# Attention, gated MLP and routed experts on one core: where the softmax is divided, and which engine takes the low parts

## The reference

```python
scores = scale * np.matmul(q, k.transpose(0, 1, 3, 2))
scores = np.where(causal, -1000000000.0, scores + np.minimum(bias, 0.0))
attn = np.exp(scores - np.max(scores, axis=-1, keepdims=True))
attn = attn / (np.sum(attn, axis=-1, keepdims=True) + 1e-09)
x = np.matmul(attn, v)                       # 32 heads, then heads side by side
h = gelu(x @ w_in); u, v = halves of h       # 512 columns each
v_s = w_sg @ layernorm(v) * g_ln + b_sg      # mixes the 576 tokens of a batch
x = x + (u * v_s) @ w_out
# then each token goes to one of 8 experts: p[e] * relu(x @ w1[e]) @ w2[e]
```

## Time and profile before

| | |
|---|---|
| median of 3 runs | 983.89 us (983.05 to 987.94) |
| the profiled execution | 983.82 us, its span 981.8 us |
| turns 1 to 32, up to the last head's output | 40 to 576 us of the span |
| batch 3's MLP, routing, experts | 576 to 982 us |
| TensorE busy | 837.6 us (85%) |
| DVE, ACT, GpSimd busy | 567.6, 380.7, 379.1 us |
| mean granted TensorE clock | 0.944 |

### The profile page before, as it was taken

The page is one execution under the profiler, slowest core; times in us unless marked ns, Lnnn a source line. Parts: engine busy times, 40 slices in busy tenths (PEclk is TensorE's granted clock), DMA queues, the critical chain, the costliest instruction groups (busy, mean ns, idle before and its releaser), DMA issues.

```text
span 981.8 us, 16466 instructions
## 1 busy us (share of the span) xinstructions
PE 837.6 (85%) x5253; PEld 712.9 (73%) x5254; DVE 567.6 (58%) x1219; ACT 380.7 (39%) x862; POOL 379.1 (39%) x481
## 2 busy tenths in 40 slices
PE   2787788799978879979979999946999999999993
PEld 1566667688857768857869868926788888888773
DVE  5578647866547767546777524455664566356221
ACT  2444444533344534344434334123543244334110
POOL 1688646654545664535655430002111111111112
PEclk9989889989999989999989999965999999999997
DMA  4611101011021011020110010066353355330100
GB/s 120 184 39 43 40 13 33 14 32 32 16 79 31 15 33 31 16 79 11 36 25 14 7 49 1 1 244 249 134 207 134 126 196 211 134 124 23 44 34 23
DMA packets 81420, 70.61 MB, mean 72 GB/s; under 512 B 61960, under 2 KB 61960, under 8 KB 81322
## 3 DMA queue, kind: packets, MB, share of 16 engines
q1 hardware_dynamic: 77354, 58.49, 19.2%
q0 software_dynamic: 4000, 11.28, 3.5%
HBM read 59.72 MB, written 11.86 MB: 73 GB/s over the span
## 4 chain that ended last, share of the span: by engine, by line
PE 68%; DVE 12%; POOL 7%; ACT 7%; issue 3%; DMA 1%; POOLq 0%; DVEq 0%; ACTq 0%
PE obank L926 13%; PE sbank L1814 9%; PE sbank L1816 8%; PE sbank L1815 8%; PE sbank L1247 6%; PE sbank L1005 6%; POOL probs L510 4%; PE tbank L994 3%; PE sbank L978 3%; ACT probs L590 2%; DVE nmax L743 2%; PE sbank L980 2%; PE tbank L1005 2%; PE obank L1059 1%; POOL cube L532 1%
## 5 line engine op out<-in xcount | busy, mean ns | idle before, releaser
L510 POOL TENSOR_SCALAR probs<-probs,recip 128x128 f32<-128x128 f32 (+4 forms) x160 | 204.4, 1288 | 176.8 <-DVE recip L753 176.1
L590 ACT ACTIVATE probs<-sbank,nmax 128x128 f32<-128x128 f32 (+4 forms) x160 | 91.2, 570 | 249.2 <-DVE nmax L743 248.8
L978 PE MATMUL sbank<-k,q 128*128 128x256 f32 (+2 forms) x192 | 77.7, 410 | 63.5 <-POOL q L499 54.9
L1610 POOL DMA_INDIRECT out_dram<-y,sid x25 | 25.3, 1011 | 217.9 <-DVE y L1775 214.3
L743 DVE TENSOR_REDUCE nmax<-sbank 128x1 f32<-128x128 f32 (+4 forms) x160 | 84.7, 535 | 41.1 <-PE sbank L985 39.5
L978 PEld LDWEIGHTS sbank<-k,q 128*128 128x128 f32 x192 | 39.8, 207 | 71.8 <-issue 59.6
L994 PE MATMUL tbank<-ident,probs 128*128 128x128 f32 (+2 forms) x480 | 74.5, 278 | 5.9 <-DVE pT L759 5.4
L1005 PE MATMUL sbank<-pT,v_raw 128*64 128x128 f32 x640 | 78.2, 278 | 0.2 <-ACT pT L599 0.2
L1814 PE MATMUL sbank<-w_high,xsT_h 128*128 x184 | 74.9, 407 | 1.9 <-DVE xsT_l L1739 1.7
L1323 DVE TENSOR_TENSOR w_low<-w_low,w_high (+1 forms) x64 | 74.0, 1218 | 0.7 <-ACT w_high L1679 0.3
L1005 PEld LDWEIGHTS sbank<-pT,v_raw 128*64 128x64 f32 x640 | 70.2, 139 | 5.3 <-issue 4.2
(11 more groups left out here) (290 smaller groups left out, 2163.5 us busy)
## 6 DMA issues: line engine op xcount, KB each, us to landing
w_low<-in_moe_w_dram SPq DMA_DIRECT2D x16, 2048.0 KB, 13.3
k_raw<-in_k_dram SPq DMA_DIRECT2D x32, 128.0 KB, 2.3
q_raw<-in_q_dram SPq DMA_DIRECT2D x32, 128.0 KB, 2.4
v_raw<-in_v_dram SPq DMA_DIRECT2D x32, 128.0 KB, 2.2
x_dram<-x SPq DMA_DIRECT2D x4, 1024.0 KB, 4.3
win_raw<-in_moe_w_in_dram SPq DMA_DIRECT2D x1, 2048.0 KB, 10.7
wsg_raw<-in_moe_w_sg_dram SPq DMA_DIRECT2D x1, 1152.0 KB, 6.0
wout_raw<-in_moe_w_out_dram SPq DMA_DIRECT2D x1, 1024.0 KB, 12.8
```

The lines of the kernel that those rows point to most:

```text
L510: nc.gpsimd.tensor_scalar(w, w, recip[u][0:r, i:i + 1], None, ALU.mult).then_inc(normed, 1)
L590: nc.scalar.activation(probs_view(u, i, r), score_view(i, r), ACT.Exp, bias=nmax[u][0:r, i:i + 1], accum_out=sums[u][0:r, i:i + 1]).then_i ...
L978: nc.tensor.matmul(dst, q1[u][:, q_cols], k1[u][:, cols], start=True, stop=False)
```

## The change

- The probabilities stay as the exponentials. `turn_probs` waits for `exped`. DVE inverts the five sums of a head once, at the start of the next turn. SyncE writes the 128 x 5 reciprocals to `recip_dram`, waits for that, and reads the 576 of them back into `recipT` on 64 partitions. DVE's `output` waits for this (`recip_in`) and multiplies while it moves the head from PSUM to x. `recipT` is one buffer, so the read also waits for the output of the head before.
- `norms` is gone from GpSimd. GpSimd takes over the low parts of x for k tiles 0 to 2, of v for tiles 3 and 4, and of the gated product (`g_l`). ACT takes over `vn_h`, at points 10, 11 and 12.
- The units at points 30 and 31 are two each; x2's tiles 3 and 4 go to points 0 and 1 of the next batch (the last batch keeps four at point 31). Bank numbers come from a table of this order. DVE reads the mixing and output units one point later, and the steps behind them (g_h, g_l) move one point as well.
- The first unit of a batch and unit 13 wait piece by piece for the parts they multiply, not for all of them at the start.

```diff
+            def spread_recips(h):
+                sp.wait_ge(inverted, h + 1)
+                with nc.allow_non_contiguous_dma("small"):
+                    sp.dma_start(recip_dram[h % 2, :].rearrange("(i p) -> p i", p=P),
+                                 recip[h % 2][:, :]).then_inc(recip_out, 16)
+                sp.wait_ge(recip_out, 16 * (h + 1))
+                if h:
+                    sp.wait_ge(out_done, h)
+                sp.dma_start(recipT[:, :], recip_dram[h % 2, 0:S].rearrange("(a n) -> a n", a=1).broadcast_to([D, S])
+                             ).then_inc(recip_in, 16)
...
             for t in range(HEADS + 1):
+                if t:
+                    spread_recips(t - 1)
                 if t % 2 == 0 and t // 2 + 1 < PAIRS:
...
             def output(h):
                 dve.wait_ge(av_part, h + 1)
-                nc.vector.tensor_copy(dst[own_rows[h % 2], MAIN], O[TOP, :]).then_inc(out_part, 1)
+                dve.wait_ge(recip_in, 16 * (h + 1))
+                nc.vector.tensor_tensor(dst[own_rows[h % 2], MAIN], O[TOP, :], recipT[:, MAIN],
+                                        ALU.mult).then_inc(out_part, 1)
...
             def turn_probs(h, i, bank, at=0):
-                pe.wait_ge(normed, ST * h + i + 1)
+                pe.wait_ge(exped, ST * h + i + 1)
...
-            def norms(t, first, end):
-                pool.wait_ge(inverted, n)
-                for i in range(first, end):
-                    nc.gpsimd.tensor_scalar(w, w, recip[u][0:r, i:i + 1], None, ALU.mult).then_inc(normed, 1)
...
+                if p == 12:
+                    for m in (3, 4):
+                        pool.wait_ge(m_vnh, ST * b + m + 1)
+                        nc.gpsimd.tensor_tensor(vn_l[:, m, :], vn[:, m, :], vn_h[:, m, :].bitcast(F32),
+                                                ALU.subtract).then_inc(m_vnl_pool, 1)
...
+                    if p in (10, 11, 12):
+                        for m in ((0, 1), (2, 3), (4,))[p - 10]:
+                            act.wait_ge(m_norm, ST * b + m + 1)
+                            nc.scalar.copy(vn_h[:, m, :], vn[:, m, :]).then_inc(m_vnh, 1)
...
-            first = POINTS - 3
-            return {first: [LOGITS, LOGITS + 1], first + 1: [TILES, TILES + 1, TILES + 2],
-                    first + 2: [TILES + 3, TILES + 4, TURN]}[p]
+            if p < 2 and b:
+                here.append((b - 1, TILES + 3 + p))
+            if p == POINTS - 2:
+                here = [(b, TILES), (b, TILES + 1)]
+            if p == POINTS - 1:
+                here = [(b, TURN), (b, TILES + 2)]
```

More of the change, by code:

```diff
@@ L150, in moe_block @@
         recip = [fb(f"recip{u}", [P, ST], F32) for u in range(2)]
+        recipT = fb("recipT", [D, S], F32)
         front.close()
@@ L370, in point_of @@
             return b, (s_ // 2) * 8 + (k if s_ % 2 == 0 else 5 + k)
+        places = {}
+        for b in range(B - 1):
+            for p in range(POINTS):
+                for x in units_at(b, p):
+                    places[x] = len(places)
         def number(b, n):
-            return UNITS * b + n
+            return places[b, n]
         def bank_of_unit(g):
@@ L532, in fill @@
                     nc.gpsimd.tensor_tensor(c, x, x, ALU.mult).then_inc(squared, 1)
[L533 to L538 removed]
+                    latest = squared, done + 1
@@ L546, in _ @@
-                fill(t, 0)
-                if this:
-                    norms(t, 0, 2)
-                    if even:
-                        pool.wait_ge(normed, ST * t + 2)
-                        twice(t // 2, 0, TAIL, 5)
-                        twice(t // 2, 1, TAIL, 5)
-                fill(t, 1)
-                fill(t, 2)
-                if even and this:
-                    norms(t, 2, 4)
+                first_x = even and t >= HPB and t % HPB == 0
+                latest = fill(t, 0, latest)
@@ new lines, in _ @@
+                if this and even:
+                    pool.wait_ge(*latest)
+                    twice(t // 2, 0, TAIL, 5)
+                    twice(t // 2, 1, TAIL, 5)
+                if first_x:
+                    latest = x_low(t // HPB - 1, 0)
+                latest = fill(t, 1, latest)
+                if first_x:
+                    latest = x_low(t // HPB - 1, 1)
+                latest = fill(t, 2, latest)
+                if first_x:
+                    latest = x_low(t // HPB - 1, 2)
@@ L827, in fill @@
                     if p in (11, 12):
-                        for m in (range(0, 3), range(3, ST))[p - 11]:
+                        for m in ((0,), (1, 2))[p - 11]:
                             dve.wait_ge(m_vnh, ST * b + m + 1)
@@ L865, in fill @@
                         nc.vector.tensor_copy(logit[:, b, :, :], src[:, :, 0:E + 1]).then_inc(emptied[g % 2], 1)
-                if t % HPB == 0 and t >= HPB and k < 3:
-                    x_low(t // HPB - 1, k)
             for u in range(2):
@@ L1095, in fill @@
                     pe.wait_ge(misc_in, 48)
-                for n in units_at(p):
-                    unit(b, n)
+                for x in units_at(b, p):
+                    unit(*x)
             pe.wait_ge(pool_own, 5)
```

172 lines of the change are left out of this document (91 added, 81 removed).

## The result

The changed kernel takes **1057.22 us** (median of four runs, 1055.15 to 1060.13) against 983.89: a ratio of 1.074, 95% interval 1.070 to 1.078. The forecast was 944, the range 926 to 968. The fourth rival, "DVE stands at the round trip", is what happened.

What follows compares the result with a forecast made beforehand. TensorE was taken as the bound, with holes and some time at 1.2 GHz. Batches 32.7 and 6, early turns 4.3 and 5, together 48, less 8.5, gave 39.5 us off 983.8: 944 us, range 926 to 968.

Steps and rivals of the forecast that it cites:

- DVE stands at the round trip: Rival: DVE waits at output, turns last at least the trip plus 3.2 us; 1,031 us at a 15 us trip; chance 0.07.
- What is added: Costs of the new output and DMAs: multiplying costs nothing, round trip 5.5 us; charges -3.5, -1.5 and -3.5 us.
- The charge for the loop: Loop of output, row maximum, exponential, inversion and round trip: 0.5 us charged seven times in shortened turns, -3.5 us.
- Turns 2 to 8: Early even turns' starting wait shrinks 0.4 us each, 1.6 us; half the early clock loss returns, 5 us.
- Tiles of x2: Turns 16 and 24: the third tile's wait for a bank ACT empties goes, 3.7 us in two batches, 7.4 us.
- First unit of a batch: Nine matmuls can go before the awaited fourth low part, saving 2.0 us a batch, 6.0 us.
- The last exponential: TensorE's 5.0 us wait for ACT's last exponential halves as DVE loses two of three inversions a turn, 2.5 us.
- Start of turns 10, 18, 26 and of 12, 20, 28: GpSimd's copies of k and q come sooner: 6.6 us at the first three starts, 10.2 us at the others.
- Unit 13: At turns 12, 20, 28 it meets its parts piecemeal; GpSimd's last two low parts cost it some 0.7 us.
- No difference: Rival: DVE waits for reciprocals as long as TensorE waited for GpSimd, trip near 12 us; 979 to 989 us; chance 0.05.
- The chain moves to ACT: Rival: ACT's casts of v delay the next k and q, unit 13 starts no earlier; 965 us; chance 0.22.
- More holes close: Rival: the clock holds nearly throughout, returning 15 of the other 17 us of clock loss; 929 us; chance 0.06.

Runs made afterwards that it cites:

- e4: Changed kernel writing only the first column of reciprocals, 128 neighbouring elements of 4 bytes, and reading ones instead; 1037.1 us.
- e3: Changed kernel with its 640 writes of 4 bytes put 512 bytes apart, and reading ones instead; 949.2 us.
- e9: Changed kernel with reciprocals written as 128 rows of 20 bytes and DVE reading them with a step of five; 950.93 us, ratio 0.967.
- e1: Changed kernel without the two DMAs of the reciprocals and DVE's wait for them, multiplying by a constant 1.0; 943.64 us, ratio 0.956.
- e7: Changed kernel's units, bank order and low parts, but the old division with GpSimd multiplying the probabilities; 959.10 us, ratio 0.974.
- e10: Kernel before with only the reciprocals' part of the change, written as 128 rows of 20 bytes; 969.15 us, ratio 0.986.
- e11: As e9, but the reciprocals are written three times, one write after another, for a trip of 9.3 us; 982.7 us, ratio 0.995.
- e5: Separate kernel of single DMAs, no layers, varying element distance and order; 640 elements in the change's order, 4 to 32 bytes apart: 8.6 to 2.2 us.
- e6: Changed kernel without DMAs of reciprocals: ones beside v put row sums in the product and DVE inverts them there; 1055.47 us, ratio 1.072.

## Why the prediction was wrong

**The step that failed** is the first number of *What is added*: "In bytes it is nearest to the load; I take 5.5", with bounds of 4.6 and 6.5. Measured: 12.7. The lower bound came from reads of 4-byte elements, the upper from one big write; neither is a write of 4 bytes beside another's 4 bytes. The text even said that no row shows such a write, and then closed the range at the next rows. The upper bound was no bound. Bytes were the wrong measure of nearness: e4, with 0.5 KB, takes 8.1 us where 2.5 KB take 8.6, and e3, with the same 2.5 KB, a quarter of it. The estimate of 4 us that stands beside it, from the Trainium skill (DMA: Bandwidth & Descriptors, the anatomy of one DMA), was lower still. That section is about DMAs that GpSimd issues, these are SyncE's, and even the fast trip takes 5.1.

A second step failed with it: "this is mostly hidden", and the loop of the trip plus 3.2 us charged to short turns only. Heads with odd numbers have the longer loop, since their inversion stands behind the next head's first row maximum: trip plus 7.0 us or more.

**The sum without that step nearly held.** The forecast of 944 includes 5.0 us for a trip of 5.5; e9, with a trip of 5.1, has 950.9, a gain of 33 where 39.5 was forecast. Without the 5.0 it is 939; e1, without a trip, has 943.6. Term by term, before against e9 or e1:

- *The charge for the loop*, -3.5 for a trip of 5.5 us, and *turn 1*, -1.5. Together 5.0 forecast; e9 is 5.8 behind e1 at the last output of the profiled executions, 7.3 by the medians of the whole. The shares were the other way round: 4.4 in turns 0 and 1, little in the loop.
- *Turn 0*, 2.7: the first output moves from 40.05 to 37.56 in e1, 2.5.
- *Turns 2 to 8*, 1.6 and 5 for the clock: 89.1 to 83.9 us in e1, 5.2 for 6.6. The clock hardly rose (0.89 to 0.90), and TensorE's busy time fell by 2.7 of the 5.
- *The batches*, 32.7 plus 6 for the clock less 3.5: net 35.2. Measured 446.7 to 413.4 in e9, 33.3. By the windows of e9 below TensorE's busy time falls 3.0 of the 6, and its idle time from 56.5 to 26.1, that is 30.4, for 32.7 less 3.5.

```profile
41.97:127.78 85.81, 71.30 (x494) 59.13 (x495) 61.23 (x133) 42.70 (x123) 25.03 (x51) 0.82 0.25 54
127.78:541.16 413.38, 387.27 (x2823) 337.67 (x2821) 262.90 (x564) 199.97 (x527) 114.52 (x174) 0.97 0.18 42
```

Inside the batches the terms were less good than their sum. TensorE's waits in e9, from 127.78 to 541.16, answer to the earlier trace rows:

```profile
PE obank L963 <- DVE vn_l L876: 7.1, 6, 1.6
PE sbank L1015 <- POOL q L531: 5.6, 5, 1.6
PE tbank L1031 <- DVE pT L800: 5.3, 5, 1.6
...
PE obank L1115 <- ACT x L694: 2.2, 2, 1.1
...
PE obank L963 <- DVE x_l L817: 0.7, 3, 0.3
```

- *Tiles of x2* (8.2 us of wait, 7.4 taken) leaves 2.2; *First unit of a batch* (8.6, 6.0 taken) leaves 0.7; *The last exponential* (5.0, 2.5 taken) is gone. These three gave 18.9 us of wait, not 15.9.
- *Start of turns 10, 18, 26 and of 12, 20, 28.* The wait for GpSimd's q goes from 28.6 to 5.6, by 23.0, more than the terms' 16.8 plus the 2.1 charged for unit 13. But the stretches from head 8's to head 11's output and their like in the other batches, which hold both starts, shrink by 13.6 in all (190.4 to 176.8), 3 less than 16.8. Nearly all of it, 12.3, is in their first two intervals, with the starts of turns 10, 18 and 26, for which 6.6 was forecast. The lengths up to the outputs of heads 11, 19 and 27, in which the holes of 7 us lay, go only from 76.3 to 75.0, where 10.2 was forecast.
- *Unit 13*, "cost the unit some 0.7 us". It waits 7.1 us in six pieces, 2.4 a batch, and not for GpSimd's parts but for DVE's.

Why unit 13 waits shows in e9's timeline at the start of turn 12:

```profile
183.63 0.36 PE L1015 MATMUL sbank<-k,q 128*128 128x256 f32 x1 [1.61 <-POOL q L531]
...
184.17 3.16 POOL L561 TENSOR_TENSOR vn_l<-vn,vn_h 128x512 fp32r<-128x512 f32 x2
184.45 3.43 DVE L876 TENSOR_TENSOR vn_l<-vn,vn_h 128x512 fp32r<-128x512 f32 x2
...
186.25 0.61 PE L963 MATMUL obank<-wsg_h,vn_h 128*128 128x288 f32 x1 [1.63 <-DVE vn_l L876]
...
187.93 0.61 PE L963 MATMUL obank<-wsg_h,vn_h 128*128 128x288 f32 x1 [0.60 <-DVE vn_l L876]
```

GpSimd's low parts take 1.58 us each, not 1.04, the row of the square that the prediction used. DVE's two at the same time take 1.71 each, where the same instruction takes 0.74 and 0.68 a few microseconds earlier (179.43). In e7, where the two engines' subtractions do not meet, GpSimd's take 1.27. So using both engines at once gives next to nothing here: two of DVE at 0.68 and two of GpSimd at 1.27 are 3.9 us one after the other, and the two pairs together take 3.7. All four on DVE would be an estimated 2.7. (e10 leaves them on DVE; unit 13 waits 5.3 us in it.)

The Trainium skill (SBUF — State Buffer, Who interferes with whom) says that a VectorE instruction with two inputs in SBUF and a GpSimd instruction that reads SBUF exclude each other; the trace agrees in that the 3.43 us above are two and a half times 1.36 (two of 0.68), though it records both engines as slower and shows neither as blocked. The Trainium skill's rule that the prediction weighed (GPSIMD Engine Reference, section 3.1, Elementwise: twice DVE's time) gave 1.5 us; the 1.27 of e7 lie midway between that and the square's row, and beside DVE it is 1.58.

The clock is at 0.50 from 185.72 to 192.55; it fell within the second of three pauses of 1.6, 1.6 and 0.6 us. In this stretch TensorE is busy 5.7 us, an estimated 2.8 more than at 1.00. The pauses and this together, 6.7 us, are nearly the 7.2 of the one pause before.

**The rivals.** *Slower: DVE stands at the round trip* was right in its mechanism: DVE's idle time before `output` ends at a DMA in 30 of 32 heads, as "Wrong:" had it, and the short turns last the trip plus 3.0 us or more. It was wrong in its place and price. It put break-even at a trip of 12 us and 1,031 at 15; measured, break-even lies between 9.3 (e11, still 0.5% faster) and 12.7, by the curve an estimated 10 or just under, and the time is 1,057 at 12.7. It let only short turns pay. Against e1 the outputs with even numbers, nearly all of them short intervals, come 62 us later in sum, those with odd numbers 42, and the first 10: 114. And it priced no clock: of the 104 us beyond the first output, 39 are TensorE's own work getting slower (busy 86.6 for 66.7 and 407.1 for 388.0) and 65 are idle. Its chance of 0.07 hung on the trip's bounds; with 640 unpriced writes in the loop that was too little. *No difference* had 979 to 989 for a trip near 12; the 1,057 at 12.7 answers it. *The chain moves to ACT*: no run shows unit 13 held by ACT's casts. *More holes close*: the clock in the early turns stayed at 0.90 even without a trip.

## What to carry to other kernels

A write of a few kilobytes was priced here by how its pieces lie at the destination, not by its bytes or their number. Two ways were fast: each partition writes its values as one row, and the order is undone where they are read; or single values are 32 bytes or more apart in the change's order. Before a DMA goes into a loop between engines, find every chain behind it (here also the transposes that shared banks with the waiting product) and everything that the engine's program puts ahead of the instruction that starts it (here a row maximum of the next head). Then compute the longest trip that each turn can hold, the long turns included. And where no row prices an operation, the nearest rows are no upper bound: say what happens at twice the price, and give that case its weight.

## What was unexpected of the hardware

- 640 writes of 4 bytes side by side land in 8.6 us, 32 bytes apart in 2.2, as rows of 20 bytes in 1.8 (e5); 128 of them side by side take 8.1 (e4). The five values of a row 64 bytes from one another still take 2.9 (e5).
- Values that were written so directly before are read in 4.4 us instead of 2.9 (e5).
- DVE's reciprocal takes 3359 ns for 64x512 from PSUM (e6), 6.6 ns for each of the 512 columns, where a copy takes 682 in all.
- A second input with a step of five elements makes DVE's multiplication of 64x512 take 1082 instead of 684 ns (e9).
- DVE's and GpSimd's subtractions of 128x512 beside each other take 1.7 and 1.6 us (e9), for 0.7 of DVE (e9) and 1.3 of GpSimd (e7) apart.
